# Three weight loads are issued before the last y stores have landed, and the y staging buffer changes its place

## The chip, the cores and the metric

The kernel runs on one core of one Trainium2 chip. Its time is the device time of one execution in microseconds (us). A core has five engines that run their own instruction streams: TensorE (PE in the profile) multiplies matrices, VectorE (DVE), ScalarE (ACT) and GpSimd (POOL) work on elements, SyncE (SP) only issues transfers. POOL issues transfers too. The transfers of both run on the core's 16 DMA engines. The streams are tied together by semaphores alone.

## The reference, cut to what matters

Attention in chunks of 32 queries over 8 memory rows and a context of up to 56 rows gives 3072 tokens of 512 values. Two blocks of fully connected layers follow:

```
h = max(x @ w1, x @ w2, x @ w3)          # 512 -> 768
y = h @ w_out                            # 768 -> 512
u = y @ w_in2                            # 512 -> 2048
g = u if u >= 1, 0 if u <= -1, else (u + 1)**2 / 4
out = g @ w_out2                         # 2048 -> 512
```

## The kernel before

Every product of the layers is made of three matmuls, since each operand is split into a high part and a rest: high by high, rest by high, high by rest (lines 449 to 451).

The first half (attention and the first block) works on 8 tiles of 384 tokens. The y of a tile is made in four blocks d = 0 to 3 of 128 columns (`layer2`). ACT copies a block's high part from PSUM into `y_stage` (`y_out`, line 637), DVE puts the rest beside it (`y_low`, line 805), and SP stores both in DRAM, in `y_scratch` (`store_y`, line 238, semaphores `y_stored[0]` for even d and `y_stored[1]` for odd d). `y_stage` has two places, so block d waits until the store of block d - 2 has landed.

The second half works on 12 tiles of 256 tokens. `up` makes a pair p of column blocks of u (24 matmuls), ACT and DVE turn it into g, and `down` multiplies g by the weights of `w_out2` (21 matmuls; seven products on sums of blocks in place of eight products). The sums of the weights were made in the first half and lie in DRAM (`wc_scratch`). There are eight of them, p = 0 to 7, of 1792 KB each, and they are loaded once, by POOL, into `wc[:, p]` (`load_wc`, line 371). The y of a tile comes in two loads of 512 KB (`load_y`, line 379) into `y0` or `y1` by turns.

On PE the first tile of the second half runs `up` for pairs 0 to 7, and `down` of pair p - 2 after `up` of pair p. Each of these `down` waits for its own `wc_in[p]`. The last two, `down` of pairs 6 and 7, fall into the second tile, which is inside a loop. So PE waits for `wc_in[6]` and `wc_in[7]` once, ahead of the loop, after `down` of pair 5.

The tensors of the second half lie over those of the first half. With an offset in bytes per partition that follows from the order of allocation:

- `w_in2_hi`, `w_in2_lo` and `wc[0]` lie over attention's buffers, `stage_a` and the first part of `w123_hi`
- `wc[1]` to `wc[5]` lie over `w123_hi`, `w123_lo`, `x1_hi` and `x1_lo`
- `wc[6]` and `wc[7]` lie over the end of `x1_lo` and over `w_out1_hi` and `w_out1_lo`
- `g_hl`, slot 1, and `out_a` lie over the end of `h_max` and over `y_stage`

This is why POOL loads in steps. It issues `wc[0]` when layer 1 of the last tile is done. It issues `wc[1]` after the store of y block 0 of that tile has landed, and `wc[2]` after that of block 1. It issues `wc[3]` to `wc[5]` after those of blocks 2 and 3, the y of tile 1 when the last matmul of the first half is done, and then `wc[6]` and `wc[7]`. ACT, for its part, waits for the last y stores before it first writes slot 1 of `g_hl`. POOL and ACT take their instructions strictly in order.

Of the kernel before, what the change touches and what calls it, by code (L numbers as in the profile page):

```python
# [8 lines left out]
F32R = mybir.dt.float32r  # L9
# [17 lines left out]
TT = 384  # L27
GPT = TT // P
TOKENS = B * S
TILES = TOKENS // TT  # L30
# [19 lines left out]
def build_attention_and_two_mlps(nc, qk_l, v_l, w123, w_out1, w_in2, w_out2, out):  # L50
# [9 lines left out]
    with ExitStack() as ctx:  # L60
# [3 lines left out]
        def sem(name):  # L64
            return ctx.enter_context(nc.semaphore(name))

        def sbuf(where, name, shape, dt=F32):
            return where.enter_context(nc.sbuf_tensor(name, [P, *shape], dt))
# [13 lines left out]
        phase_a = ExitStack()  # L82
# [10 lines left out]
        w123_lo = sbuf(phase_a, "w123_lo", [KF1, 3 * KD, P], F32R)  # L93
        x1_hi = sbuf(phase_a, "x1_hi", [KD, TT], F32R)
        x1_lo = sbuf(phase_a, "x1_lo", [KD, TT], F32R)
        w_out1_hi = sbuf(phase_a, "w_out1_hi", [KF1 * DM], F32R)
        w_out1_lo = sbuf(phase_a, "w_out1_lo", [KF1 * DM], F32R)
        h_hi = sbuf(phase_a, "h_hi", [KF1, TT], F32R)
        h_lo = sbuf(phase_a, "h_lo", [KF1, TT], F32R)
        h_part = sbuf(phase_a, "h_part", [TT])  # L100
        h_max = sbuf(phase_a, "h_max", [2, TT])
        y_stage = sbuf(phase_a, "y_stage", [2, 2, TT], F32R)
        phase_a.close()


# [58 lines left out]
        y_stored = [sem(f"y_stored{i}") for i in range(2)]  # L164
# [18 lines left out]
        AHEAD = 1  # L183
# [136 lines left out]
        def _(pool):  # L320
# [49 lines left out]
            def load_wc(p):  # L370
                pool.dma_start(wc[:, p].rearrange("p h c -> p (h c)"), wc_scratch[p]).then_inc(wc_in[p], 16)

            def load_y(u):

                tiles = (TB * (u + 1) - 1) // TT + 1
                for s in y_stored:
                    pool.wait_ge(s, 16 * AHEAD + 32 * tiles)
                for h in range(2):
                    pool.dma_start(y_of[u % 2][:, h], y_scratch[h, :, :, TB * u:TB * (u + 1)]).then_inc(y_in[u % 2], 16)
# [6 lines left out]
            for d in range(2):  # L386
                pool.wait_ge(y_stored[d], 16 * AHEAD + 32 * (TILES - 1) + 16)
                load_wc(1 + d)
            for s in y_stored:
                pool.wait_ge(s, 16 * AHEAD + 32 * TILES)  # L390
            for p in range(3, 6):
                load_wc(p)
            pool.wait_ge(mlp_done, TG * TILES)
            load_y(1)
            load_wc(6)
            load_wc(7)
            for u in range(2, TILES_B):
# [198 lines left out]
        def _(act):  # L596
            def copy(o, i):
                return act.activation(o, i, ACT.Copy)  # L598
# [101 lines left out]

            def raw_high(g, p):
                act.wait_ge(g_done, g + 1)
                if isinstance(g, int) and g < 2:
                    if g == 1:

                        act.wait_ge(y_stored[0], 16 * AHEAD + 32 * TILES)
                        act.wait_ge(y_stored[1], 16 * AHEAD + 32 * TILES)
                else:
                    act.wait_ge(down_done, g - 1)
                copy(g_hl[:, p % 2, 0, G_SUMS:].rearrange("p (x q) -> p x q", x=2),  # L710
                     g_f32[:, p % 2].rearrange("p (x q) -> p x q", x=4)[:, 0:4:3]).then_inc(g_hi_done, 1)
# [18 lines left out]
            def tile_b(u, first=False):  # L730
                for p in range(PAIRS):
                    g = PAIRS * u + p
                    ramp(g, p)
                    if p == 1 and not first:
                        drain(u - 1)
                    raw_high(g, p)
                    sums_high(g, p)
# [216 lines left out]
```

## Time and profile before

| | |
|---|---|
| device time, median of 3 runs | 1012.54 us (1012.16 to 1013.75) |
| device time of the profiled execution | 1010.6 us |
| its span, first to last instruction | 1008.8 us |
| PE busy | 988.1 us, 98% of the span |
| DVE, ACT, POOL busy | 505.8, 378.4, 131.0 us |
| mean granted TensorE clock | 0.997 of full speed |
| DMA moved | 107.93 MB, mean 107 GB/s |

A busy PE is one that has a matmul in it; the share says nothing on the clock at which it ran. Each row of the timeline begins with the start in us from the span's start and the duration of one instruction. Matmuls overlap, so the time that one costs is the distance between two starts. Text in brackets gives the idle time of the engine before the instruction and what ended it.

### The profile page before, as it was taken

Reading aid. Unit: us, or ns where it says so; the run is one execution under the profiler, and the core shown is the slowest. Engines: PE = TensorE matmul, PEld = TensorE weight load, DVE = VectorE, ACT = ScalarE, POOL = GpSimd, SP = SyncE. Lnnn points to the kernel's source line nnn. Section 1 sums busy time; section 2 is a strip of 40 time slices with the busy share of each in tenths; the row PEclk is TensorE's granted clock in tenths of the full one; section 3 lists DMA queues with packets and bytes.
Section 4 is the critical chain, followed back from the end, with each engine's and each line's share of the span. In section 5 each row is a group of like instructions: output and inputs, shape, how many; then the busy total and the mean of one; then the engine's idle time right before and its main releaser. Section 6 shows DMA issues by size and latency. Waiting matters only on the chain.

```text
span 1008.8 us, 22903 instructions
## 1 busy us (share of the span) xinstructions
PE 988.1 (98%) x9792; PEld 975.2 (97%) x9792; DVE 505.8 (50%) x1011; ACT 378.4 (38%) x645; POOL 131.0 (13%) x128
## 2 busy tenths in 40 slices
PE   5999999999999999999989999999999999999997
PEld 4999999999999999999989999999999999999997
DVE  4663434354343424322546556565665656556564
ACT  3342222222221222251434444454454544544453
POOL 1123306152320000062100000000000000000000
PEclk9999999999999999999999999999999999999999
DMA  9453555273635320065880102101020210102000
GB/s 365 169 209 121 194 182 207 96 260 110 226 126 188 106 84 2 32 199 155 344 273 22 43 22 62 42 21 42 21 62 3 60 42 21 42 21 62 0 22 22
DMA packets 41793, 107.93 MB, mean 107 GB/s; under 512 B 2817, under 2 KB 29441, under 8 KB 39681
## 3 DMA queue, kind: packets, MB, share of 16 engines
q1 hardware_dynamic: 27904, 79.70, 22.0%
q0 software_dynamic: 13824, 27.27, 9.0%
q8 instruction: 54, 0.88, 0.4%
q14 instruction: 11, 0.08, 0.0%
HBM read 73.40 MB, written 33.55 MB: 106 GB/s over the span
## 4 chain that ended last, share of the span: by engine, by line
PE 94%; DMA 4%; DVE 1%; issue 1%; ACT 0%; POOL 0%; DVEq 0%; POOLq 0%
PE mlp L449 20%; PE mlp L451 20%; PE mlp L450 20%; PE scores_ps L451 4%; PE scores_ps L450 4%; PE scores_ps L449 4%; PE attn_ps L449 4%; PE attn_ps L451 4%; PE attn_ps L450 4%; PE attn_ps L442 3%; DMA wc<-wc_scratch 2%; PE scores_ps L418 2%; DMA y_scratch<-y_stage 1%; PE trans_ps L451 1%; PE trans_ps L450 1%; PE trans_ps L449 1%
## 5 line engine op out<-in xcount | busy, mean ns | idle before, releaser
L449 PE MATMUL mlp<-x_hi,w_hi 128*128 128x384 f32 x576 | 197.2, 342 | 1.6 <-issue 1.6
L451 PE MATMUL mlp<-x_lo,w_hi 128*128 128x384 f32 x576 | 193.3, 336 | 0.0
L450 PE MATMUL mlp<-x_hi,w_lo 128*128 128x384 f32 x576 | 193.1, 335 | 0.0
L449 PE MATMUL mlp<-y,w_in_hi 128*128 128x256 f32 x576 | 163.7, 284 | 3.1 <-DMA wc<-wc_scratch 3.1
L451 PE MATMUL mlp<-y,w_in_hi 128*128 128x256 f32 x576 | 163.7, 284 | 0.0
L450 PE MATMUL mlp<-y,w_in_lo 128*128 128x256 f32 x576 | 163.7, 284 | 0.0
L449 PEld LDWEIGHTS mlp<-y,w_in_hi 128*128 128x128 f32 x576 | 111.1, 193 | 3.3 <-issue 3.3
L856 DVE SCALAR_TENSOR_TENSOR g_f<-g_f,mlp 128x512 f32<-128x512 f32 x72 | 49.4, 686 | 127.4 <-ACT g_f L699 127.4
L449 PEld LDWEIGHTS mlp<-x_hi,w_hi 128*128 128x128 f32 x576 | 108.6, 188 | 3.6 <-issue 1.7
L451 PEld LDWEIGHTS mlp<-y,w_in_hi 128*128 128x128 f32 x576 | 111.3, 193 | 0.0
L450 PEld LDWEIGHTS mlp<-y,w_in_lo 128*128 128x128 f32 x576 | 111.2, 193 | 0.0
L450 PE MATMUL scores_ps<-wc,g_hl 128*128 128x256 f32 x384 | 108.7, 283 | 0.0
L451 PE MATMUL scores_ps<-wc,g_hl 128*128 128x256 f32 x384 | 108.7, 283 | 0.0
L449 PE MATMUL scores_ps<-wc,g_hl 128*128 128x256 f32 x384 | 108.7, 283 | 0.0
L450 PEld LDWEIGHTS mlp<-x_hi,w_lo 128*128 128x128 f32 x576 | 108.7, 189 | 0.0
L451 PEld LDWEIGHTS mlp<-x_lo,w_hi 128*128 128x128 f32 x576 | 108.5, 188 | 0.0
L875 DVE TENSOR_TENSOR g_hl<-g_sums,g_hl 128x640 fp32r<-128x640 f32 x96 | 79.1, 824 | 36.4 <-ACT g_hl L598 36.4
L697 ACT ACTIVATE g_f<-mlp,half_col 128x512 f32<-128x512 f32 x72 | 49.5, 687 | 112.6 <-PE mlp L451 112.6
L598 ACT ACTIVATE h_hi<-h_max 128x384 fp32r<-128x384 f32 x48 | 25.1, 524 | 168.3 <-DVE h_max L796 168.3
L598 ACT ACTIVATE g_hl<-g_f 128x256 fp32r<-128x256 f32 x96 | 40.2, 419 | 104.8 <-PE scores_ps L451 84.2
L598 ACT ACTIVATE g_hl<-g_sums 128x640 fp32r<-128x640 f32 x96 | 70.9, 739 | 17.0 <-DVE g_sums L867 9.7
L790 DVE TENSOR_TENSOR h_max<-h_part,mlp 128x384 f32<-128x384 f32 x48 | 26.6, 554 | 95.0 <-PE mlp L451 95.0
(97 smaller groups left out, 2047.7 us busy)
## 6 DMA issues: line engine op xcount, KB each, us to landing
qk_raw<-qk_l SPq DMA_DIRECT2D x24, 768.0 KB, 8.0
wc_scratch<-stage_a SPq DMA_DIRECT2D x8, 1792.0 KB, 8.6
wc<-wc_scratch POOLq DMA_DIRECT2D x8, 1792.0 KB, 11.5
v_raw<-v_l SPq DMA_DIRECT2D x24, 512.0 KB, 4.4
y_scratch<-y_stage SPq DMA_DIRECT2D x32, 384.0 KB, 2.5
y<-y_scratch POOLq DMA_DIRECT2D x24, 512.0 KB, 4.9
stage_a<-w SPq DMA_DIRECT2D x6, 768.0 KB, 6.9
stage_b<-w_out SPq DMA_DIRECT2D x8, 512.0 KB, 7.0
```

The costliest lines, as they stand in the source:

```text
L418: last = pe.matmul(scores_v[part, r, i], q[rows, i, part], k[rows, i, c], start=True, stop=True)
L442: last = pe.matmul(attn_o[r * D:(r + 1) * D, i, m, c], v_raw[rows, j, 2 * m + r, c], prob_t[rows, 2 * m + r, c], start=True, stop=True)
L449: pe.matmul(out_ap, a_hi, b_hi, start=first, stop=False, skip_group_check=beside)
L450: pe.matmul(out_ap, a_lo, b_hi, start=False, stop=False, skip_group_check=beside)
L451: return pe.matmul(out_ap, a_hi, b_lo, start=False, stop=last, skip_group_check=beside)
L598: return act.activation(o, i, ACT.Copy)
L697: act.activation(g_f32[:, p % 2], mlp[p % MLP_BANKS], ACT.Relu, bias=half_col[:, 0:1], scale=0.5).then_inc(ramp_done, 1)
L790: dve.tensor_tensor(h_max[:, f % 2], h_part[:, :], mlp[1][:, 0:TT], ALU.max).then_inc(h_max2_done, 1)
L856: dve.scalar_tensor_tensor(g_f32[:, p % 2], g_f32[:, p % 2], 1.0, mlp[p % MLP_BANKS], ALU.min, ALU.max).then_inc(g_done, 1)
L875: dve.tensor_tensor(g_hl[:, p % 2, 1, 0:G_SUMS], g_sums[:, :], g_hl[:, p % 2, 0, 0:G_SUMS].bitcast(F32), ALU.subtract).then_inc(g_split, 1)
```

## The change

`y_stage` is allocated right after `x1_lo` and not at the end. `w_out1`, `h`, `h_part` and `h_max` move up by its 6144 bytes per partition. It then lies under `wc[6]`, and no longer under `g_hl` and `out_a`. The wait for the last two y stores moves in POOL's stream from ahead of `wc[3]` to ahead of `wc[6]`, and the wait in ACT's stream is dropped.

```
--- before.py
+++ after.py
@@ -93,13 +93,13 @@
         x1_hi = sbuf(phase_a, "x1_hi", [KD, TT], F32R)
         x1_lo = sbuf(phase_a, "x1_lo", [KD, TT], F32R)
+        y_stage = sbuf(phase_a, "y_stage", [2, 2, TT], F32R)
         w_out1_hi = sbuf(phase_a, "w_out1_hi", [KF1 * DM], F32R)
         w_out1_lo = sbuf(phase_a, "w_out1_lo", [KF1 * DM], F32R)
         h_hi = sbuf(phase_a, "h_hi", [KF1, TT], F32R)
         h_lo = sbuf(phase_a, "h_lo", [KF1, TT], F32R)
         h_part = sbuf(phase_a, "h_part", [TT])
         h_max = sbuf(phase_a, "h_max", [2, TT])
-        y_stage = sbuf(phase_a, "y_stage", [2, 2, TT], F32R)
         phase_a.close()
@@ -386,12 +386,12 @@
             for d in range(2):
                 pool.wait_ge(y_stored[d], 16 * AHEAD + 32 * (TILES - 1) + 16)
                 load_wc(1 + d)
-            for s in y_stored:
-                pool.wait_ge(s, 16 * AHEAD + 32 * TILES)
             for p in range(3, 6):
                 load_wc(p)
             pool.wait_ge(mlp_done, TG * TILES)
             load_y(1)
+            for s in y_stored:
+                pool.wait_ge(s, 16 * AHEAD + 32 * TILES)
             load_wc(6)
             load_wc(7)
@@ -700,12 +700,7 @@
             def raw_high(g, p):
                 act.wait_ge(g_done, g + 1)
-                if isinstance(g, int) and g < 2:
-                    if g == 1:
-
-                        act.wait_ge(y_stored[0], 16 * AHEAD + 32 * TILES)
-                        act.wait_ge(y_stored[1], 16 * AHEAD + 32 * TILES)
-                else:
+                if not isinstance(g, int) or g >= 2:
                     act.wait_ge(down_done, g - 1)
```

POOL's stream where the two halves meet, before the change. The rows with `wc` are the loads of pairs 0 to 7 in order, those with `y` the loads of the y of tiles 0, 1 and 2:

```order
L379 DMA y<-y_scratch 128x4x256
L371 DMA wc<-wc_scratch 128x3584 [waits mlp_done,wc_stored]
L371 DMA wc<-wc_scratch 128x3584 [waits y_stored0]
L371 DMA wc<-wc_scratch 128x3584 [waits y_stored1]
L371 DMA wc<-wc_scratch 128x3584 [waits y_stored1,y_stored0]
L371 DMA wc<-wc_scratch 128x3584 x2
L379 DMA y<-y_scratch 128x4x256 [waits y_stored1,y_stored0,mlp_done]
L379 DMA y<-y_scratch 128x4x256
L371 DMA wc<-wc_scratch 128x3584 x2
L379 DMA y<-y_scratch 128x4x256 [waits y_stored1,y_stored0,up_done]
```

And with the change:

```order
L379 DMA y<-y_scratch 128x4x256
L371 DMA wc<-wc_scratch 128x3584 [waits mlp_done,wc_stored]
L371 DMA wc<-wc_scratch 128x3584 [waits y_stored0]
L371 DMA wc<-wc_scratch 128x3584 [waits y_stored1]
L371 DMA wc<-wc_scratch 128x3584 x3
L379 DMA y<-y_scratch 128x4x256 [waits y_stored1,y_stored0,mlp_done]
L379 DMA y<-y_scratch 128x4x256
L371 DMA wc<-wc_scratch 128x3584 [waits y_stored1,y_stored0]
L371 DMA wc<-wc_scratch 128x3584
L379 DMA y<-y_scratch 128x4x256 [waits y_stored1,y_stored0,up_done]
```

The loads of pairs 3 to 5 now follow that of pair 2 without a wait, and so does the y of tile 1, whose wait on `y_stored` asks for earlier tiles only. The full wait stands ahead of pair 6.

ACT's stream for the second pair (g = 1) of the first tile of the second half; `g_hl` from `g_f` is the row of `raw_high`:

```order
-L598 ACTIVATE g_hl<-g_f 128x256 [waits y_stored1,y_stored0,g_done]
-L598 ACTIVATE g_hl<-g_sums 128x640 [waits sums_done]
-L697 ACTIVATE g_f<-mlp,half_col 128x512 [waits up_done]
-L699 ACTIVATE g_f<-g_f 128x512 [waits ramp_done]
-L598 ACTIVATE g_hl<-g_f 128x256 [waits down_done,g_done]
+L598 ACTIVATE g_hl<-g_f 128x256 [waits g_done]
+L598 ACTIVATE g_hl<-g_sums 128x640 [waits sums_done]
+L697 ACTIVATE g_f<-mlp,half_col 128x512 [waits up_done]
+L699 ACTIVATE g_f<-g_f 128x512 [waits ramp_done]
+L598 ACTIVATE g_hl<-g_f 128x256 [waits down_done,g_done]
```

Only the first row's list of waits is shorter. PE's, DVE's and SP's streams hold the same instructions in the same order.

## Rows read from the trace of the kernel before

**Rows 1.** The page's first lines: span, and busy time of the engines.

```profile
span 1008.8 us, 22903 instructions
PE 988.1 (98%) x9792; PEld 975.2 (97%) x9792; DVE 505.8 (50%) x1011; ACT 378.4 (38%) x645; POOL 131.0 (13%) x128
```

**Rows 2.** Timeline of PE around 518 us: start, duration, instruction, idle before.

```profile
517.78 0.28 PE L451 MATMUL scores_ps<-wc,g_hl 128*128 128x256 f32 x1
521.19 0.38 PE L449 MATMUL mlp<-y,w_in_hi 128*128 128x256 f32 x1 [3.13 <-DMA wc<-wc_scratch]
```

**Rows 3.** Chain of waits that ended last, 470 to 540 us: start, duration, what.

```profile
480.92 10.71 DMA y_scratch<-y_stage
491.67 0.47 issue
...
495.71 24.93 DMA wc<-wc_scratch
520.63 0.56 issue
```

**Rows 4.** Stretches: PE, PEld, DVE, ACT, POOL busy; clock; DMA share; GB/s.

```profile
521.19:526.39 5.20, 5.20 (x31) 5.20 (x31) 0.00 (x0) 0.62 (x1) 0.00 (x0) 0.67 0.18 33
567.00:610.20 43.20, 43.20 (x362) 43.20 (x362) 25.57 (x55) 21.05 (x36) 1.47 (x2) 1.00 0.13 35
```

**Rows 5.** Timeline of POOL, 476 to 516 us: the issues of wc and y loads.

```profile
477.37 0.54 POOL L371 DMA_DIRECT2D wc<-wc_scratch  x1 [9.00 <-DMA y_scratch<-y_stage]
478.35 0.53 POOL L371 DMA_DIRECT2D wc<-wc_scratch  x1 [0.44 <-DMA y_scratch<-y_stage]
492.13 1.59 POOL L371 DMA_DIRECT2D wc<-wc_scratch  x3 [13.26 <-DMA y_scratch<-y_stage]
493.69 1.49 POOL L379 DMA_DIRECT2D y<-y_scratch  x2
495.17 1.08 POOL L371 DMA_DIRECT2D wc<-wc_scratch  x2
```

**Rows 6.** Issues at 477.37, 478.35, 492.13, 493.17, 495.17 us: count, KB, us to landing.

```profile
wc<-wc_scratch POOLq DMA_DIRECT2D x1, 1792.0 KB, 7.5
...
wc<-wc_scratch POOLq DMA_DIRECT2D x1, 1792.0 KB, 12.0
...
wc<-wc_scratch POOLq DMA_DIRECT2D x1, 1792.0 KB, 7.3
...
wc<-wc_scratch POOLq DMA_DIRECT2D x1, 1792.0 KB, 15.8
...
wc<-wc_scratch POOLq DMA_DIRECT2D x1, 1792.0 KB, 21.1
```

**Rows 7.** Stretches as in rows 4: the gap between loads, and a full stretch.

```profile
491.00:494.50 3.50, 3.50 (x30) 3.41 (x29) 1.70 (x3) 2.25 (x4) 2.37 (x5) 1.00 0.39 80
498.50:506.00 7.50, 7.50 (x65) 7.50 (x64) 4.93 (x11) 4.71 (x8) 0.00 (x0) 1.00 1.05 436
```

**Rows 8.** DMA queues, 482.5 to 489 us: packets, MB, share of 16 engines.

```profile
q0 software_dynamic: 176, 2.29, 90.6%
q1 hardware_dynamic: 174, 0.27, 13.0%
```

**Rows 9.** DMA queues, 489 to 491.7 us, when q0 is nearly empty.

```profile
q1 hardware_dynamic: 370, 0.52, 52.1%
q0 software_dynamic: 18, 0.03, 3.4%
q8 instruction: 1, 0.02, 2.2%
```

**Rows 10.** DMA queues, 471.56 to 474 us, after the issue of a y store.

```profile
q0 software_dynamic: 68, 0.97, 103.1%
q8 instruction: 1, 0.02, 2.4%
```

**Rows 11.** Timeline of ACT: the first write of g_hl's slot 1.

```profile
491.73 0.42 ACT L598 ACTIVATE g_hl<-g_f 128x256 fp32r<-128x256 f32 x1 [3.97 <-DMA y_scratch<-y_stage]
```

**Rows 12.** Timeline of PE: last matmul of a block of u, first of down.

```profile
493.52 0.28 PE L451 MATMUL attn_ps<-y,w_in_hi 128*128 128x256 f32 x1
493.69 0.39 PE L449 MATMUL attn_ps<-wc,g_hl 128*128 128x256 f32 x1
```

More of the change, by code:

```diff
@@ L95, in build_attention_and_two_mlps @@
         x1_lo = sbuf(phase_a, "x1_lo", [KD, TT], F32R)
+        y_stage = sbuf(phase_a, "y_stage", [2, 2, TT], F32R)
         w_out1_hi = sbuf(phase_a, "w_out1_hi", [KF1 * DM], F32R)
@@ L101, in build_attention_and_two_mlps @@
         h_max = sbuf(phase_a, "h_max", [2, TT])
-        y_stage = sbuf(phase_a, "y_stage", [2, 2, TT], F32R)
         phase_a.close()
@@ L388, in _ @@
                 load_wc(1 + d)
-            for s in y_stored:
-                pool.wait_ge(s, 16 * AHEAD + 32 * TILES)
             for p in range(3, 6):
@@ L394, in _ @@
             load_y(1)
+            for s in y_stored:
+                pool.wait_ge(s, 16 * AHEAD + 32 * TILES)
             load_wc(6)
@@ L702, in raw_high @@
                 act.wait_ge(g_done, g + 1)
[L703 to L708, printed above, removed]
+                if not isinstance(g, int) or g >= 2:
                     act.wait_ge(down_done, g - 1)
```

## The prediction, made before the changed kernel was run

> **What bounds the kernel now.** I read the page first. PE is busy for 988.1 of 1008.8 us [rows 1], so nothing counts but gaps in PE's stream and stretches in which it runs slowly. Next I read what PE waited for. After the start-up of the first 28 us, which the change does not touch, there is one gap: the matmul before it starts at 517.78, the one behind it at 521.19, and what ended the gap is a load of wc [rows 2]. In the steady stretch a tile of 8 x (24 + 21) = 360 matmuls takes 43.20 us [rows 4], 0.12 us each. So the next matmul was due at 517.90, and it came 3.29 us late. Third, the granted clock behind the gap: 0.67 on average from 521.19 to 526.39 [rows 4], which is partly the lower level (1.2 GHz) and partly the upper (2.4 GHz). In that stretch PE did the 24 matmuls of an `up` and 6 of the `down` behind it, in 5.20 us. At 0.12 they take 3.60. The low clock cost another 1.60 us. The place costs 4.89 us in all.
>
> Fourth, the chain of waits shows where the gap comes from. The last y store is issued at 480.92 and lands after 10.71 us. POOL goes on 0.47 us later, and its last load, pair 7, takes 24.93 us to land at 520.63. PE starts 0.56 us behind that [rows 3]. POOL stood for 13.26 us ahead of pair 3 [rows 5]. From the issues [rows 5] and the times to landing [rows 6] the loads of pairs 1, 2, 3, 5 and 6 land at 484.9, 490.4, 499.4, 509.0 and 516.3, in the order of issue. They wait for bandwidth, not for each other: 436 GB/s flow from 498.5 to 506, but only 80 from 491 to 494.5 [rows 7]. That trough is what the wait on the y stores costs.
>
> **The change, part by part.**
>
> *The wait on POOL.* It removes nothing that is moved. All bytes go over the same 16 DMA engines; the trough is filled. Pairs 3 to 5 are issued from about 478.9 (the end of the issue at 478.35 [rows 5]), at 0.53 each, and the two y loads behind them at 0.75 each, done at about 482. Seven transfers were outstanding at 496 as well, without an issue that took longer, so I price the depth of the queue at nothing.
>
> When does pair 7 land? I start at the landing of pair 2, 490.4, which nothing ahead of it changes. Pair 3 follows directly, at the distance of pair 7 from pair 6, 520.63 - 516.3 = 4.3 us. From pair 3 to pair 7 the trace has 499.4 to 520.6 = 21.2 us, with pairs 4 to 7 and the y of tile 1 in it. That gives 490.4 + 4.3 + 21.2 = 515.9. To this comes what is left of the last two y stores, which now have to pass among the loads. They are 544 packets; 174 have gone by 489, one for each of 176 packets of the loads [rows 8]; at that rate 35 more by 490.4. 335 are left. Priced by the mixed stretch they take 13.0% of 6.5 us for 174, so 1.6 us for 335. Priced by the stretch in which they ran alone (370 in 2.7 us [rows 9]) they take 2.4 us. The landing is 517.5 to 518.3; I take 518.1, nearer to the upper end, since a fetch of instructions (16 KB, 2.2% of 16 engines in 2.7 us, which is 0.95 us of one engine [rows 9]) fell into the trough before and now falls among the loads. If it falls on the engine that is last anyway, it adds 0.95: 519.1. The lower end is set by the full rate: 5 loads of 1.835 MB, y of 1.05 MB and 0.51 MB of stores are 10.7 MB, at 436 GB/s 24.6 us, so 515.0.
>
> *The wait on POOL ahead of pair 6.* At one packet of the store for each packet of the loads, 335 packets of stores need 335 of the loads, and a load has 144 (128 and 16 for its semaphore). That is 2.3 loads: the stores land in the load of pair 5, near 502 or 503. POOL issues pair 6 about 0.5 us later, while pair 5 and the y of tile 1 still flow until about 508. So the queue does not run dry, and this wait costs nothing. Behind it on POOL stand pairs 6 and 7 alone; the y of tile 2 is asked for at 516 anyway.
>
> *The waits of the earlier `down`.* Pair 1 is wanted at 493.69 [rows 12], the others each 45 x 0.12 = 5.4 us later: pair 2 at 499.1, 3 at 504.5, 4 at 509.9, 5 at 515.3. In one queue they now land at about 484.9, 490.4, 495.7, 501 and 506. Each has 8 us to spare. The y of tile 1 lands near 510, against 518.
>
> *The wait on ACT.* ACT stood 3.97 us [rows 11], and the `down` of pair 1 hangs on it: it starts 0.17 us after the matmul before it, in place of 0.12, and the first one runs long (0.39 [rows 12]); the loss is 0.05 to 0.15 us. It goes. PE then reaches its wait for pairs 6 and 7 at about 517.8.
>
> *The new place of `y_stage`.* The same instructions on other addresses. In the rows nothing depends on an address; cost 0, and I know of no row to bound it.
>
> *The sum.* Pair 7 lands at 518.1, PE starts at 518.7 and not at 521.19: -2.5 us. The gap shrinks from 3.29 to about 0.9 us. Does the clock still fall behind it? No row shows a gap between 0.2 and 3.1 us at the full clock. The fall costs between 0 and 1.60 us. A gap of 0.9 is nearer to the tiny ones, behind which the clock stays at 1.00, so I take 0: -1.6. The sum is -4.1 us. At the best (landing by 517.2) all of it goes: 4.89 + 0.15 = -5.0.
>
> The profiled execution took 1010.6 us, 1.8 more than its span. It becomes 1006.5. It is 1.9 below the median of the runs, 1012.54, from which I count: 1012.54 - 4.1 = 1008.4.
>
> **Where the skill and the rows differ.** The loads ran at 436 GB/s in a full stretch [rows 7]. The Trainium skill ("DMA: Bandwidth & Descriptors", section "Where 436 GB/s comes from") says that for transfers between HBM and SBUF the HBM side binds, at about 358 GB/s. By that rule the 10.7 MB would take 30 us, pair 7 would land at 520.4, and the change would bring nothing; the row has a higher rate for 7.5 us on end, so I do not follow it. The stores' packets pass one for one with those of the loads [rows 8]. The same page (section "Queues, rings and completion order") says that a DMA engine takes a whole packet, typically of 9 to 17 descriptors, from one ring before it turns to the next. By that the stores would be done after two turns, long before 502, and the chance that pair 6 is issued late would be zero; the sum stays.
>
> **The rivals.**
>
> *No gap at all.* The loads keep nearer to the full rate and pair 7 lands by 517.2. For it: the bound of 515.0. Against it: the observed 21.2 us for 8.4 MB is only 395 GB/s. -5.0 us: 1007.5.
>
> *The gap is short, but the clock falls.* For it: it fell behind the one gap that there is. Against it: this one is less than a third as long. -2.5 us: 1010.0.
>
> *The rate is worse than in my sum.* 10.2 MB took from about 493.4 to 520.6, 375 GB/s with the start. At this rate the 10.7 MB take 28.6 us, pair 7 lands at 519.0; with the instruction fetch on the last engine at 520. PE starts at 519.6 to 520.5, and the clock falls: -0.7 to -1.6. About 1011.4.
>
> *The stores starve.* After the issue of a store at 471.56 not one of its packets passed until 474 while a load was running [rows 10]. If q1 waits until q0 is empty, the loads run on unmixed until about 505, the stores land near 508, and pair 7 needs 0.47 + 7.3 + 4.3 = 12.1 us more: 520. Against it: rows 8. It gives -0.7; it turns into a loss only if the last store lands after 508.5.
>
> *Slower.* With five loads in one queue at once the engines could share it among them and not serve it in order. All would then land near 490.4 + 3 x 4.3 = 503, and PE would stand at the `down` of pair 1 from 493.6 to 503, 9.5 us, with 1.60 for the clock; the 4.9 of the later gap go: +6.2, 1018.7. It decides where the new gap and its clock outweigh the old 4.9: once the gap is over 3.3 us, so once pair 1 lands after 493.1 + 3.3 = 496.4. Against it: in the second batch five loads stood together and landed 4 to 7 us apart in order.
>
> **How the numbers follow.** Forecast 0.43, no gap 0.20, clock falls 0.14, worse rate 0.12, starving stores 0.06, slower 0.05. 0.2% is 2.0 us, about what a measurement of this kernel can tell from no change. The first three are beyond it: faster 0.77; the next two are within: same 0.18; slower 0.05. The range runs from the best case with half a us for the scatter of the runs, 1006.8, up to 1011.4, the worse rate. Above it lie the starving stores, a part of the worse rate, and the slower case.
>
> **What would show it.** In the changed profile POOL issues wc three times right behind 478.9 and waits for the y store ahead of pair 6, until 502 or 503 (much earlier: the stores did not pass one for one; 507 or later: they starved). There is no trough near 492. ACT no longer waits for y_scratch. Pair 7 lands at 518.1, and PE's gap ahead of the loop is 0.9 us or less, with the clock at 1.00 behind it. A clock of 0.5 there is the second rival. A PE gap at 493.6 or 499 would make the prediction wrong in kind, and a landing after 520 in size.

## The result and the profile after

| | before | changed |
|---|---|---|
| runs compared | 1012.17 us median of 5 (1011.75 to 1013.75) | 1006.43 us median of 5 (1006.34 to 1007.35) |
| ratio, 95% interval | | 0.9944, 0.9932 to 0.9955 |
| again, both run once more on another chip | 1011.65 us median of 10 (1010.01 to 1012.06) | 1006.71 us median of 5 (1006.58 to 1007.10) |
| ratio, 95% interval | | 0.9955, 0.9942 to 0.9969 |
| profiled execution, span | 1010.6 us, 1008.8 us | 1007.35 us, 1005.6 us |

By the two ratios the change makes the kernel 4.6 to 5.7 us faster (the repeat was expected near 0.995). I had forecast 4.1 us and a time between 1006.8 and 1011.4; the time lies 0.4 us below that range.

In the changed kernel POOL's stream reads as forecast: four loads of wc (pairs 2 to 5) stand together, and the wait is ahead of pair 6. Timeline of POOL, to be read against [rows 5]:

```profile
479.55 0.54 POOL L371 DMA_DIRECT2D wc<-wc_scratch  x1 [9.70 <-DMA y_scratch<-y_stage]
480.54 2.11 POOL L371 DMA_DIRECT2D wc<-wc_scratch  x4 [0.45 <-DMA y_scratch<-y_stage]
482.62 1.49 POOL L379 DMA_DIRECT2D y<-y_scratch  x2
505.36 1.07 POOL L371 DMA_DIRECT2D wc<-wc_scratch  x2 [21.25 <-DMA y_scratch<-y_stage]
```

POOL stands for 21.25 us and not for 13.26 [rows 5], and this costs nothing, because the queue is full the while. Stretches of the changed kernel, with the columns of [rows 4]; the last one is the GB/s:

```profile
491.00:494.50 3.50, 3.50 (x31) 3.50 (x30) 2.58 (x6) 2.36 (x4) 0.00 (x0) 1.00 1.06 419
494.50:498.50 4.00, 4.00 (x36) 4.00 (x35) 3.08 (x8) 2.41 (x5) 0.00 (x0) 1.00 1.04 414
498.50:506.00 7.50, 7.50 (x65) 7.50 (x64) 3.97 (x8) 3.17 (x5) 0.64 (x2) 1.00 1.04 410
```

Where 80 GB/s flowed [rows 7] there are now 419. The y stores pass one for one with the loads nearly all the way. DMA queues, 489 to 502 us, which answers to [rows 8]:

```profile
q0 software_dynamic: 382, 4.80, 89.1%
q1 hardware_dynamic: 383, 0.56, 13.8%
```

The counts are as even in a short piece. From 489.72 to 490.28 us each of the 16 DMA engines took about one packet of the loads, in 0.55 us, and one of the stores:

```profile
q0 software_dynamic: 16, 0.23, 98.0%
q1 hardware_dynamic: 15, 0.02, 13.2%
```

The last store was issued at about 482.4 and took 22.4 us to land, in place of 10.7 [rows 3]. Pair 7 was issued at 505.9 and took 13.0 us, so it landed at 518.9. Pair 2, issued at 480.54, landed at 492.0. Issues in the order of pair 2, the store, pair 7:

```profile
wc<-wc_scratch POOLq DMA_DIRECT2D x1, 1792.0 KB, 11.5
...
y_scratch<-y_stage SPq DMA_DIRECT2D x1, 384.0 KB, 22.4
...
wc<-wc_scratch POOLq DMA_DIRECT2D x1, 1792.0 KB, 13.0
```

And PE ahead of its loop, which answers to [rows 2]. The two matmuls stand 0.35 us apart, not 3.41:

```profile
519.12 0.28 PE L451 MATMUL scores_ps<-wc,g_hl 128*128 128x256 f32 x1
519.47 0.38 PE L449 MATMUL mlp<-y,w_in_hi 128*128 128x256 f32 x1
```

**Where the time went between the two profiles.** I cut both at three points: the first matmul of the second half, the first behind the loop's start, and ACT's first copy of `out_a`. First before, then changed:

```profile
25.00:31.00 6.00, 6.00 (x87) 5.66 (x87) 1.38 (x2) 1.03 (x3) 3.48 (x1) 1.00 0.19 55
479.62:521.19 41.57, 38.44 (x319) 38.15 (x319) 23.29 (x49) 19.74 (x33) 5.61 (x9) 1.00 1.05 371
521.19:532.52 11.33, 11.33 (x82) 11.33 (x83) 2.90 (x6) 3.70 (x6) 0.00 (x0) 0.85 0.08 15
```

```profile
25.00:31.00 6.00, 6.00 (x81) 5.39 (x82) 0.87 (x2) 0.69 (x2) 3.46 (x1) 1.00 0.24 59
481.09:519.47 38.38, 38.31 (x319) 38.11 (x319) 21.55 (x46) 18.82 (x31) 5.59 (x9) 1.00 1.02 384
519.47:529.29 9.82, 9.82 (x82) 9.82 (x83) 4.54 (x10) 4.85 (x8) 0.00 (x0) 1.00 0.35 89
```

The first tile of the second half is 41.57 - 38.38 = 3.19 us shorter. Of these 3.06 are the gap (3.41 less 0.35 us between the two matmuls), and 0.13 lie ahead of it, about what I had given ACT's wait. The next stretch is 11.33 - 9.82 = 1.51 us shorter, the clock (0.85 before, 1.00 now). Together 4.70.

The first rows show why the spans differ by 3.2 only. In the changed kernel's profiled execution PE did 81 matmuls from 25 to 31 us and not 87, and the second half began 1.47 us later, at 481.09 and not at 479.62. The clock column reads 1.00 in both rows and does not show the difference. The matmuls do: at the start of the kernel they stand 0.32 us apart and later 0.17, and the pace doubles later in the changed kernel. First before, then changed:

```profile
27.35 0.39 PE L451 MATMUL mlp<-x_lo,w_hi 128*128 128x384 f32 x1
27.58 0.33 PE L449 MATMUL mlp<-x_hi,w_hi 128*128 128x384 f32 x1
27.75 0.33 PE L450 MATMUL mlp<-x_hi,w_lo 128*128 128x384 f32 x1
```

```profile
28.10 0.52 PE L450 MATMUL mlp<-x_hi,w_lo 128*128 128x384 f32 x1
28.42 0.52 PE L451 MATMUL mlp<-x_lo,w_hi 128*128 128x384 f32 x1
...
30.45 0.34 PE L450 MATMUL mlp<-x_hi,w_lo 128*128 128x384 f32 x1
30.62 0.34 PE L451 MATMUL mlp<-x_lo,w_hi 128*128 128x384 f32 x1
```

This has nothing to do with the change: over the profiles of all the kernels here the second half begins between 479.6 and 481.2, at 479.99 in a variant with the changed kernel's loads (experiment 6) and at 480.69 in the second profile of the kernel before. 4.70 - 1.47 = 3.23.

### The profile page after: what moved, and what is told of

Read it like the earlier page. It is cut to its first block, busy times and chain, and to the rows that moved or that the text cites. A ratio compares the mean times of both kernels' runs of the same rounds, so it can differ in the third digit from the quotient of the medians.

```text
span 1005.6 us, 22902 instructions
## 1 busy us (share of the span) xinstructions
PE 987.9 (98%) x9792; PEld 974.7 (97%) x9792; DVE 506.8 (50%) x1011; ACT 378.1 (38%) x645; POOL 131.2 (13%) x128
## 4 chain that ended last, share of the span: by engine, by line
PE 98%; DVE 1%; DMA 0%; issue 0%; ACT 0%; DVEq 0%
PE mlp L449 21%; PE mlp L451 20%; PE mlp L450 20%; PE attn_ps L449 5%; PE attn_ps L451 5%; PE attn_ps L450 5%; PE scores_ps L450 5%; PE scores_ps L451 5%; PE scores_ps L449 5%; PE attn_ps L442 3%; PE scores_ps L418 2%; PE trans_ps L451 1%; PE trans_ps L450 1%; PE trans_ps L449 1%; PE trans_ps L425 1%; DMA qk_raw<-qk_l 0%
## 5 line engine op out<-in xcount | busy, mean ns | idle before, releaser
L449 PEld LDWEIGHTS scores_ps<-wc,g_hl 128*128 128x128 f32 x384 | 73.7, 192 | 0.0
```

What stands on the lines that cost most here:

```text
L449: pe.matmul(out_ap, a_hi, b_hi, start=first, stop=False, skip_group_check=beside)
```

## The experiments

**1. The kernel before, once more (before_again).** No edit. It was run because the medians (5.7 us) and the cut above (4.7) did not agree.

> The kernel before, unchanged, with span and granted clock of every run. What is asked: the change brought 5.7 us by the medians, but only 3.2 us between the two profiled executions, and in the profile its place accounts for 4.7. Theory A (the low clock behind the gap has no fixed length): the runs of this kernel scatter over 2 to 3 us, the slower ones have a mean granted clock lower by 0.001 to 0.002 than the profile of before (0.997), and another profile shows more than 3.4 us at the lower level behind the gap in at least some executions. Theory B (the start-up alone scatters): all runs have the same mean clock of 0.997 behind the start-up, the scatter is below 1.7 us as with the changed kernel, and the 1 us that is left over is chance. Median 1012.2 by both.

Measured: 1012.46 us median of 12 (1011.24 to 1013.34); beside it 29 runs of the same kernel, 1011.59 (1010.31 to 1014.48); ratio 0.9999, 0.9988 to 1.0009. The profile has a gap of 3.2 us, and the lower clock over 6.8 us, not 3.4:

```profile
521.13:527.94 6.81, 5.55 (x26) 5.56 (x27) 0.27 (x1) 0.03 (x1) 0.00 (x0) 0.50 0.45 86
```

The clock fell here at 521.1, while PE still stood in the gap, and behind the gap 5.5 us went by at the lower level. Theory A holds. All 69 executions of this kernel with a mean clock on record in this study, on three chips, taken together:

| mean granted clock | executions | median us | from, to |
|---|---|---|---|
| 0.999 | 8 | 1010.4 | 1009.95, 1011.6 |
| 0.998 | 16 | 1011.3 | 1010.12, 1012.52 |
| 0.997 | 24 | 1011.5 | 1010.91, 1012.27 |
| 0.996 | 21 | 1013.3 | 1012.45, 1014.48 |

A loss of 0.001 in the mean is 2 us at half the clock, and so 1 us of PE's time. A stretch of 3.4 us at the lower level costs 0.0017 of the mean, one of 6.8 us 0.0034. The mean is not a clean measure, since it also counts the end of the span, where PE has nothing left to do. In the changed kernel:

```profile
1003.30:1005.50 2.20, 0.00 (x0) 0.00 (x0) 0.00 (x0) 0.00 (x0) 0.00 (x0) 0.50 0.39 134
```

In the profiles this end takes 0.7 to 3.4 us, so 0.0004 to 0.0017 of the mean, and costs nothing. So an execution at 0.996 has 6.8 us at the lower level like this profile, one at 0.997 has 3.4, one at 0.999 has none, and at 0.998 it can be 3.4 or none. Only one of the 69 has a profile, so this is read from the means, but the profiles of this study agree: 0.997 with 3.4 us behind the gap (three of them), 0.995 or 0.996 with 6.8 (three), 0.998 to 1.000 with none (five). The profile that I had read [rows 4] was of the middle kind.

**2. The new place alone (layout_only).**

```
+        y_stage = sbuf(phase_a, ...)     # behind x1_lo
-        y_stage = sbuf(phase_a, ...)     # at the end
         # waits of POOL and ACT as before
```

> The new place of y_stage alone, both waits where they were. The theory that the trough in the loads is the whole cause: 1012.2, no change, the same gap of 3.1 us ahead of the loop. The rival that the addresses matter: a gain of 0.5 us or more.

Measured: 1011.78 us (1009.56 to 1013.39, 12 runs), ratio 0.9992, 0.9981 to 1.0003; a gap of 3.3 us. No change, as by the first theory. A gain of 0.5 us (0.9995) is inside the interval, so it is the gap in the profile, not the time, that speaks against the rival.

**3. The new place and ACT's wait dropped (act_only).**

```
                 act.wait_ge(g_done, g + 1)
-                if isinstance(g, int) and g < 2:
-                    if g == 1:
-                        act.wait_ge(y_stored[0], 16 * AHEAD + 32 * TILES)
-                        act.wait_ge(y_stored[1], 16 * AHEAD + 32 * TILES)
-                else:
+                if not isinstance(g, int) or g >= 2:
                     act.wait_ge(down_done, g - 1)
```

> The new place of y_stage and the wait on ACT dropped, the loads as before. My sum gave the wait on ACT 0.05 to 0.15 us of PE's time, and since PE then reaches the wait ahead of the loop earlier without pair 7 landing earlier, none of it should be seen: 1012.2, the gap longer by that 0.1. The rival that the ACT wait is a part of the gain by itself: 1011.5 or less.

Measured: 1012.21 us (1009.83 to 1014.44, 12 runs), ratio 0.9994, 0.9983 to 1.0004. No change. Its profiled execution is the slowest of the 12, and its gap is 5.4 us:

```profile
524.77 0.58 PE L449 MATMUL mlp<-y,w_in_hi 128*128 128x256 f32 x1 [5.42 <-DMA wc<-wc_scratch]
```

POOL was let go at 495.75 there, 15.28 us into its wait, though most of the last store's 16 parts had landed by 493.1; one part came at 495.2. From 493.2 to 495.3 the queues moved the last two packets of the store and a fetch of instructions of 16 KB:

```profile
q8 instruction: 1, 0.02, 2.9%
q1 hardware_dynamic: 2, 0.00, 0.6%
```

The fetch took 0.97 us from 493.25, and the store's last 1.5 KB followed at 494.20. That it held the store up is likely and not shown. So with the old order a store that is late by 2 us goes straight into the gap.

**4. The early loads with ACT's wait kept (loads_only).** The changed kernel with the lines that experiment 3 removes put back:

```
-                if not isinstance(g, int) or g >= 2:
+                if isinstance(g, int) and g < 2:
+                    if g == 1:
+                        act.wait_ge(y_stored[0], 16 * AHEAD + 32 * TILES)
+                        act.wait_ge(y_stored[1], 16 * AHEAD + 32 * TILES)
+                else:
```

> The new place of y_stage and the early loads, but ACT still waits for the last y stores before slot 1 of g_hl. If the two parts were independent, as my sum had them, this would be 0.15 us slower than the changed kernel: 1006.6. Theory: they are not. With five loads in the queue the last store lands at about 504 and not at 491.7, so ACT stands until then and PE stands at the down of pair 1 from about 494 to 506, 12 us, and 1.6 for the clock; pair 7 has landed by then. 1006.4 + 13.5 = 1020, slower than before by 8.

Measured: 1019.34 us (1018.45 to 1019.89, 6 runs), ratio 1.0061, 1.0049 to 1.0073: 6.2 us slower than before by the ratio, 7.8 by the medians (1011.59 for the 29 runs beside it), and 12.9 slower than the changed kernel's median. ACT's wait is 14.89 us long in place of 3.97 [rows 11], and PE stands 10.8 us at the `down` of pair 1:

```profile
503.77 0.42 ACT L598 ACTIVATE g_hl<-g_f 128x256 fp32r<-128x256 f32 x1 [14.89 <-DMA y_scratch<-y_stage]
```

```profile
L449 PE MATMUL attn_ps<-wc,g_hl 128*128 128x256 f32 x3 | 1.3, 427 | 10.8 <-DVE g_hl L875 10.8
```

The theory holds. The early loads delay the last y store by 11 us here (21.6 us to land, not 10.7), and who waits for that store decides the sign of the change.

**5. PE's wait moved, loads as before (use_wait_before2).**

```
-            pe.wait_ge(wc_in[PAIRS - 2], 16)      # ahead of the loop
-            pe.wait_ge(wc_in[PAIRS - 1], 16)
             ...
-                if isinstance(u, int) and u == 0:
+                if p >= PAIRS - 2 or (isinstance(u, int) and u == 0):
                     pe.wait_ge(wc_in[p], 16)      # in down(u, p)
```

> The kernel before, with the loads as they were, but PE waits for pairs 6 and 7 at the down that reads them, inside the loop, and no longer ahead of it. Theory (the gap ahead of the loop and the low clock behind it are all that the change took away): pair 7 lands at 521 to 522 as before, the down of pair 6 wants its weights 2.9 us after the loop's start and that of pair 7 5.4 us later, both behind the landing. The gap is gone with the trough still there, and the time is that of the changed kernel, 1006.4 to 1006.9. The rival that the early loads bring something beside the gap (less contention, ACT's wait): it stays 0.5 us or more above the changed kernel.

Measured: 1006.89 us (1006.49 to 1007.64, 5 runs), ratio 0.9947, 0.9934 to 0.9960. This is the changed kernel's gain within the scatter, with the trough still there: POOL waited 13.53 us for the y store, as before. Pair 7, issued at 497.7, took 25.0 us and landed at 522.6, 2.8 us after PE had begun the loop without a gap (POOL, then PE):

```profile
494.08 1.58 POOL L371 DMA_DIRECT2D wc<-wc_scratch  x3 [13.53 <-DMA y_scratch<-y_stage]
```

```profile
519.74 0.28 PE L451 MATMUL scores_ps<-wc,g_hl 128*128 128x256 f32 x1
519.86 0.28 PE L449 MATMUL mlp<-y,w_in_hi 128*128 128x256 f32 x1
```

So the trough costs nothing by itself that these runs can tell. The gap ahead of the loop and the clock behind it are the whole of the gain, to within a few tenths of a us. ACT's late write shows too: PE is idle for 0.47 us ahead of the matmul at 495.63, which starts 0.74 us behind the one before it and not 0.12.

**6. The same in the changed kernel (use_wait_after2).**

> The changed kernel with the same move of PE's wait. In the changed kernel the matmul ahead of the loop and the one behind it stand 0.35 us apart in place of 0.12, with pair 7 landed 0.56 us before the second. If that is still a wait for pair 7, the 0.23 us go here: 1006.2 and a distance of 0.12. If it is the entry into the loop, the distance stays 0.35.

Measured: 1006.59 us (1005.93 to 1007.11, 5 runs), ratio 0.9947, 0.9934 to 0.9960. The distance ahead of the loop is 0.12 us:

```profile
518.02 0.28 PE L451 MATMUL scores_ps<-wc,g_hl 128*128 128x256 f32 x1
518.14 0.28 PE L449 MATMUL mlp<-y,w_in_hi 128*128 128x256 f32 x1
```

That alone doesn't show what the 0.23 us were. In the second profile of the changed kernel, without this edit, the distance is 0.12 too:

```profile
518.70 0.28 PE L451 MATMUL scores_ps<-wc,g_hl 128*128 128x256 f32 x1
518.82 0.38 PE L449 MATMUL mlp<-y,w_in_hi 128*128 128x256 f32 x1
```

So it is not the entry into the loop, which costs nothing there. The 0.23 us of the first profile were still a wait for pair 7, which had landed 0.56 us before the matmul, as in the kernel before [rows 3]; in the second profile pair 7 is just in time. They are too few to be told in the time: no version here is measurably faster than the changed kernel.

**7 to 9. What a gap does to the clock.** Three kernels, each the changed one with a later issue of pairs 6 and 7:

```
+            pool.wait_ge(square_done, 6)   # gap_square; g_done: gap_gdone2; g_split: gap_split2
             load_wc(6)
             load_wc(7)
```

> The changed kernel with pairs 6 and 7 issued when the sixth square is done (about 508.1). Pair 7 lands 12.1 us later at 520.2, a gap of about 1.4 us ahead of the loop. Behind a gap of 2.1 us the clock fell in 3 of 7 executions, behind 3.2 us in most. Theory (the chance of a fall grows with the gap): behind 1.4 us it falls in fewer than a quarter of the executions, median 1006.4 + 1.4 = 1007.8, the few with a fall at 1009.5. The rival (a fall is a matter of moment alone, so about as frequent as with 2.1 us): nearly half of the executions at 1009.5.

> The changed kernel, with pairs 6 and 7 issued only when the sixth g is done (about 508.7), so that the DMA queue runs dry for a short time. Pair 7 lands 12.1 us behind the issue, at 520.8, and PE starts 0.56 us later: a gap of about 2.0 us ahead of the loop. What is asked is the clock: if it stays at 1.00 behind such a gap, as my forecast had it for a gap of 0.9, the time is 1006.4 + 2.0 = 1008.4 in all executions. If a gap of 2 us already lets it fall, in all executions: 1010.0. If it falls in some: a spread over 1.6 us, a median between.

> The same with the issue held until the sixth g is split (about 511.3). Pair 7 lands at 523.4: a gap of about 4.7 us. If the low stretch behind a gap has a fixed length of 3.4 us: 1006.4 + 4.7 + 1.6 = 1012.7 with the start-up's scatter of 1 us alone. If a longer gap makes low stretches of 6.8 us more frequent: a median near 1014, mean granted clocks of 0.996 or less.

| kernel | idle time of PE ahead of the loop, in its profile | median us | executions, mean clock and range of times |
|---|---|---|---|
| changed | none shown | 1006.66 (of 10) | 10 at 0.998 to 1.000, 1006.3 to 1007.4 |
| gap_square | 1.2 | 1008.09 | 6 at 0.998 to 1.000, 1007.4 to 1008.5 |
| gap_gdone2 | 2.1 | 1008.91 | 4 at 0.999, 1007.9 to 1008.9; 3 at 0.997, 1010.4 to 1010.9 |
| gap_split2 | 4.6 | 1012.65 | 8 at 0.997, 1012.4 to 1013.0; 4 at 0.996, 1013.7 to 1014.3 |

By the measure of the prediction, the distance of the two matmuls less 0.12, the four are 0.23 (0.00 in the second profile of the changed kernel), 1.32, 2.22 and 4.73 us. The gaps of the last three, from the timelines of PE, in the order of the table:

```profile
520.08 0.38 PE L450 MATMUL mlp<-y,w_in_hi 128*128 128x256 f32 x1 [1.16 <-DMA wc<-wc_scratch]
```

```profile
521.52 0.38 PE L450 MATMUL mlp<-y,w_in_hi 128*128 128x256 f32 x1 [2.06 <-DMA wc<-wc_scratch]
```

```profile
523.86 0.58 PE L450 MATMUL mlp<-y,w_in_hi 128*128 128x256 f32 x1 [4.57 <-DMA wc<-wc_scratch]
```

Behind the gap of 1.2 us the clock stayed up in all six executions; with a fall the time would be near 1009.5. Behind 2.1 us it fell in three of seven, behind 4.6 us in all twelve. This is what the theory says, that the chance grows with the gap. Against the rival for the step from 1.2 to 2.1 us it is thin: with a chance of three in seven, six executions without a fall would come about once in 29 times. In the profile of gap_gdone2 the low stretch is 3.4 us long, in that of gap_split2 6.8:

```profile
521.92:525.32 3.40, 3.40 (x18) 3.40 (x18) 0.00 (x0) 0.00 (x0) 0.00 (x0) 0.50 0.30 67
```

```profile
521.66:528.47 6.81, 4.61 (x21) 4.61 (x22) 0.00 (x0) 0.00 (x0) 0.00 (x0) 0.50 0.72 171
```

That the four at 0.996 are of the 6.8 us kind is read from this one profile and their mean clocks; there is no profile of each.

## Why the prediction was wrong

*The mechanism* was right in its steps; what missed is sizes. The wait on POOL made the trough, the trough made pair 7 late, and PE's one gap and the low clock behind it were its price. Experiments 2 and 3 show that neither the place nor ACT's wait brings anything alone, and experiment 5 reaches the same time from PE's side. The stores passed one for one and were done at 504.8 (forecast: 502 or 503), pair 6 was issued at 505.36, before the queue ran dry, and the loads landed in order. None of the rivals on starving stores, on a shared queue or on a worse rate came true. The HBM bound of 358 GB/s in "DMA: Bandwidth & Descriptors" (the Trainium skill, section "Where 436 GB/s comes from") does not bind here: 436 GB/s for the loads alone [rows 7], 410 to 419 over 15 us mixed with stores. The same page of the Trainium skill (section "Queues, rings and completion order") has a DMA engine turn from one ring to the next after a packet of typically 9 to 17 descriptors. The profile's packets are single pieces of 1.5 or 14 KB, and if each is one descriptor, the trace does not bear this out: 382 of one queue went with 383 of the other, in 0.56 us 16 with 15, and for 326 of the 367 pieces of 1.5 KB a piece of 14 KB starts just as they end.

*The first size that failed* is the landing of pair 7. I put it 27.7 us behind that of pair 2: 4.3 + 21.2 and 2.2 for the rest of the stores. Pair 2 landed at 492.0 and pair 7 at 518.9, 26.9 us; in the second profile it was 26.8. It is the 21.2 from pair 3 to pair 7, carried over from the old profile, that was too long, not the stores. From pair 2 to pair 3 (landed at 498.3) it was 6.3 us, 2.0 over the 4.3, with 176 packets of the q1 queue in it; from pair 3 to pair 7 it was 20.6 us, with 148 more in it, where the old profile had 21.2 without any; and from pair 6 to pair 7 it was 4.3 again. Why that stretch was shorter stays open. So the gap went down to 0.23 us (none in the second profile), and not to 0.9. The time came near the rival "no gap at all", with its 0.20, and not near the forecast. That is 0.7 us.

*The second* is the base. I counted from a median of three runs, 1012.54, which lay 0.8 above the median of all 69 (1011.73). Counted from that one, the forecast is 1007.6 and the range begins at 1006.0. The prediction also has 1006.5, worked out from the profiled execution (1010.6 less 4.1), and that is close to 1006.43. It is luck: the change takes 4.7 and not 4.1 from that execution, and this is made up for by its early second half, 479.62, the earliest of all the profiles.

*The third* is the clock, the term "1.60 us". I took it as a constant of the kernel, read from one execution, and it is one outcome of three: about nothing, 1.6, or two stretches. In 21 of the 69 executions, by their mean clock, it was the longest. My best case, a gain of 5.0 us, was therefore no upper bound of the gain. The changed kernel's median over 10 runs, 1006.66, is 5.1 us below that of the 69. Of this 3.2 are the gap and ACT's wait in the profiles, and 1.9 are left for the clock: 0.3 more than my 1.60. Together 0.7, 0.8 and 0.3 are the 1.8 us from 1008.4 down to 1006.66; the last is only what is left over. The range missed because it had scatter for the changed kernel only, and none for the base and for the stretch that the change takes away. Its lower end has a slip as well: the best case of 1007.5 less half a us is 1007.0, not 1006.8.

*The clock behind a short gap* was forecast to stay up behind 0.9 us. The changed kernel did not test that, but experiment 7 did, at 1.2 us: right.

*The coupling of the two edits* was missed without harm. I gave ACT's wait 0.05 to 0.15 us, and this is its price with the loads as they were (0.17 us between two matmuls in place of 0.12 [rows 12]; it varies, 0.74 us in the profile of experiment 5). With the early loads it is 12.9 us (experiment 4). I had worked out that the stores would land near 502 and not asked who else waits for them, since the change drops that wait too. Someone who had made only the first edit would have been told 1008 and got 1019.

## What to carry to other kernels

A wait ahead of a batch of transfers costs only if one of them is late for someone. Here it was the last one, and moving the transfers up or moving the wait for them down, to the instruction that reads the data, gave the same gain; the second was four lines. Before transfers are put ahead of a store in flight, list all who wait for that store: here it landed 11 to 12 us later, and the one wait left in place turned a gain of 5 us into a loss of 6 to 8. And a low clock behind a gap is a draw: here it differed from one execution to the next, so read it from the spread of the runs and not from one profile.

## What the runs showed of the hardware beyond what was expected

- The length at the lower clock behind the same gap of 3.1 to 3.3 us was 3.4 us in two profiles and 6.8 us in another. In the latter the clock fell before the gap had ended.
- The moment at which PE's pace first doubles at the start of the kernel differs too: 81 against 87 matmuls from 25 to 31 us, 1.47 us in the time of all that follows.
- With both queues full, a store of 384 KB in packets of 1.5 KB beside loads in packets of 14 KB took 22.4 us to land, one packet for one packet, against 10.7 us when the loads ended earlier. By bytes that was 0.56 MB beside 4.80 MB in 13 us.
- In experiment 4 PE stood 10.8 us, and the lower clock lasted 13.5 us and more:

```profile
497.00:510.50 13.50, 4.77 (x22) 4.77 (x23) 4.75 (x9) 4.61 (x8) 1.07 (x2) 0.50 1.18 412
```
